# A recurrence, experts and an MLP on one core: the decay scan split in four and moved, outputs turned in place of decays, activations stored transposed

## The chip, the cores and the metric

The kernel runs on one core of one Trainium2 chip, all in float32. The time is the device time of one execution in microseconds, and the number compared is the median of the runs. TensorE (PE) multiplies matrices, VectorE (DVE), ScalarE (ACT) and GpSimd (POOL) work elementwise, SyncE (SP) here issues all DMAs. Each engine has its own queue and works through it in order; semaphores tie the queues together.

## The reference

Three stages follow each other. With B = 4 batches, H = 8 heads, S = 768 tokens and D = 40 channels, the first is a recurrence over tokens with a 40x40 state for each of 32 (batch, head) pairs:

```python
for t in range(S):
    y[:, :, t] = einsum('bhd,bhde->bhe', rt, state)
    Sa = einsum('bhde,bhe->bhd', state, at)
    state = state * wt[:, :, None, :] - einsum('bhd,bhe->bhde', Sa, bt) + einsum('bhd,bhe->bhde', vt, kt)
```

Its output, as x of 4 x 768 x 320, goes through four experts, each a causal softmax attention with head size 64 (queries, keys, values, softmax, output matrix); every token takes its two best experts, weighted by a softmax over their gate logits. The last stage is an MLP: `relu(x @ w_in)` gives 1024 features, the second 512 are normalised, mixed over tokens by a 768x768 matrix with a bias, multiplied by the first 512 and brought back to 320 by `w_out`.

## The kernel before

**The recurrence** (`recurrence`, lines 26 to 1176). Tokens are cut into 24 units of 128 (4 batches of 6 blocks), a unit into 4 chunks of 32. Heads are packed: q = 0 to 3 counts pairs of heads, x = 0, 1 the head of a pair, and channels of the two heads lie at partitions 0 to 39 and 64 to 103. Within a chunk the recurrence is written in matrix form, with decays divided out: keys are multiplied by the running products of decays towards the chunk's end (`s_ch`, a backward scan over w, `scan_s`, line 970), and `a` by the running products of decays from the chunk's start (`d_ch`, `scan_d`, line 988; its start values are reciprocals that `chunk_decays`, line 979, makes out of `dc_pos`). A triangular inverse per chunk is made by repeated squaring in five levels (`level`, `level_read`, `first_power`, `grams`).

The state is carried through each chunk by three hops (`hop` on TensorE, line 874; `chain` on VectorE, line 1103). Hop 0: TensorE L892 and L898 (`a` times state) into one bank, VectorE L1110 copies it to `g_tok`. Hop 1: TensorE L908, VectorE L1118 makes `vu_tok`. Hop 2: TensorE L920, VectorE L1126 adds the state (`state_sum`), L1140 multiplies it by the next chunk's decay into `state_z`, which the next chunk's L898 reads; GpSimd L458 (`decayed_state`) makes `state`, which the next L1126 adds. Twelve hops, 4 chunks of 3, are a beat, and a beat serves one unit.

Behind every hop each engine does a piece of work for other units; what stands where is written out by hand in the functions `between` (TensorE line 800, VectorE line 1071, SP line 297) and in the loops of GpSimd (line 478) and ScalarE (line 612). In beat u, r = u + 3, t = u + 2, v = u + 1, w = u - 1 and x = u - 2 are the units worked on:

- TensorE: chunk 0: `first_grams(t)`, `turn_states(w, 0)`, `turn_decays(v)` (L662: four blocks of `d_ch`) behind hop 0; `from_values(x, 2)` and a quarter of level 1 behind hop 1, the rest of it behind hop 2. Chunk 1: `turn_values(w)` and `from_states(x, 2)`, then half of level 0 and a quarter of level 2, then the rest of level 2. Chunk 2: `grams(t, 1)`, `turn_states(w, 1)`, `r_products(w)`, then level 0 and 3. Chunk 3: `turn_keys(v)`, `from_states(w, 0)` (L784), which waits for `rvu_read`, then `from_values` and level 4.
- VectorE: `scan_s(r)` at (0,0), that is chunk 0, hop 0; `first_power(t)` (0,1); `chunk_decays(r)` and `level_read(v, 1)` (0,2); `scan_d(r)`, first half (1,0); `y_read(x)` (1,1); `scan_d(r)`, second half (1,2); `keys_of_a(t)` and `level_read(v, 2)` (2,0); `r_read(w)` (2,1), which makes `rvu` (L1058); `level_read(v, 3)` (3,0); `level_read(t, 0)` (3,1); `level_read(v, 4)` (3,2).
- GpSimd: `scaled_keys(r)` (two instructions L421, `kb_ch`, which wait for `scan_s`), `decayed_state` 0, `first_factor(t)` (L411), `sorted_decays(r)`, `decayed_state` 1, `scaled_a(r)` (L447, `a_ch`, waits for both halves of `scan_d`), `decayed_state` 2 and 3.
- ScalarE: copies of what TensorE turned (among them `decays_read`, L558, `d_tok`), `spread_power` (L510), `copy_power`, `pad_a` (waits for `a_ch`).

The outputs of a unit gather in one PSUM bank by tokens. `y_read` (L1068) multiplies them by the turned decays `d_tok` into `y_tok`, and SP stores them in 16 DMAs of 10 KB a unit (`store`, L283) into `x_dram`, laid out token by feature.

In the last three units the product of the experts' output matrix and `w_in` (`fold`, L705, 12 steps of which each third is copied by ScalarE) is put between the hops.

**Experts and MLP** (`experts_and_mlp`, line 1177). It starts when `recurrence_done` holds. For each batch n: `turn_x(n)` (L1481, L1484: 18 transposes, six groups copied alternately by VectorE, L1793, and ScalarE, L1431) makes x^T, `values_and_gates(n)` (L1501, L1505), then the MLP's hidden layer and factors of batch n - 1, `queries_and_keys(n)`, and 12 steps of attention with the dense work of batch n - 1 between. SP loads the next batch's `x_tok` once `turn_x` is through.

## Time and profile before

| what | us |
|---|---|
| median of 3 runs | 1008.67 (1002.89 to 1014.07) |
| profiled execution | 1012.26 |
| its span, first to last instruction | 1010.4 |
| last g copy (L1110) of the recurrence starts | 487.8 |
| first turn of x (L1481) starts | 501.7 |

Busy share of the span: TensorE 96%, VectorE 51%, ScalarE 46%, GpSimd 24%. The mean granted clock of TensorE was 0.978 of full speed; 1.00 is 2.4 GHz and 0.50 is 1.2 GHz. A line number such as L898 is the line of the kernel that issued the instruction. In a timeline row a figure after x is a count: a row of `x8` gives the first start and the time to the last end of eight instructions, which overlap with what follows. A bracket gives the engine's idle time ahead of the row and what ended it.

### The profile page before, as it was taken

What the parts mean: (1) busy time and instruction counts of PE and PEld (TensorE: products, weight loads), DVE (VectorE), ACT (ScalarE), POOL (GpSimd) and SP (SyncE); (2) the same over time, 40 slices, a digit from 0 to 9 for tenths busy, and PEclk for the clock granted to TensorE, in tenths of its full rate; (3) what the DMA queues carried; (4) which work ended last, traced back from release to release, by engine and by line L of the source; (5) the groups of instructions that cost most, each with busy time, mean ns of one, the idle gap of its engine ahead of it and who ended that gap; (6) DMA issues with size and microseconds to landing.
All of it is one profiled execution on the core that took longest, in us unless ns stands there. A gap on an engine that the chain in (4) does not pass through costs nothing.

```text
span 1010.4 us, 36940 instructions
## 1 busy us (share of the span) xinstructions
PE 966.7 (96%) x15708; PEld 696.7 (69%) x15708; DVE 519.6 (51%) x1443; ACT 461.7 (46%) x1122; POOL 239.0 (24%) x344
## 2 busy tenths in 40 slices
PE   6989999999999999989998999999999999999998
PEld 4878888878888888877655755567545665556555
DVE  7578777778777787744335333322343223432130
ACT  6465655555555655643227443443434424344501
POOL 8345444344344344311000000100001000110011
PEclk8599999999999999988999999999999999999999
DMA  4244344344334334241150100002000000000001
GB/s 150 63 110 112 117 118 131 90 142 126 98 99 127 96 103 130 65 128 49 36 180 2 40 1 1 1 14 66 0 1 1 21 20 0 1 1 22 19 1 39
DMA packets 51539, 63.68 MB, mean 63 GB/s; under 512 B 27440, under 2 KB 37488, under 8 KB 51376
## 3 DMA queue, kind: packets, MB, share of 16 engines
q1 hardware_dynamic: 51376, 61.32, 20.5%
q8 instruction: 125, 2.05, 0.8%
q14 instruction: 38, 0.31, 0.1%
HBM read 53.42 MB, written 7.86 MB: 61 GB/s over the span
## 4 chain that ended last, share of the span: by engine, by line
PE 82%; DVE 11%; issue 4%; ACT 2%; DMA 1%; DVEq 0%
PE banks L1628 13%; PE banks L662 7%; PE banks L726 6%; PE banks L1567 5%; PE banks L1545 4%; PE banks L1519 4%; PE banks L1596 4%; PE banks L1640 4%; PE banks L1609 4%; PE banks L1579 4%; DVE state_z L1140 4%; PE banks L908 3%; PE banks L898 3%; PE banks L773 3%; PE banks L920 2%
## 5 line engine op out<-in xcount | busy, mean ns | idle before, releaser
L510 ACT ACTIVATE powers_z<-powers,parity 128x256 f32<-128x256 f32 x240 | 108.5, 500 | 172.3 <-DVE powers L1013 172.2
L726 PE MATMUL banks<-pq,powers_z 64*64 64x64 f32 (+1 forms) x3072 | 136.6, 228 | 11.7 <-issue 5.9
L1390 POOL TENSOR_TENSOR v_st<-v_st,u_t 128x384 f32<-128x384 f32 x32 | 32.0, 999 | 473.9 <-DVE v_st L1783 473.9
L1628 PE MATMUL banks<-w_st,v_n 128*128 128x384 f32 x384 | 139.0, 496 | 0.2 <-DVE v_n L1773 0.2
L726 PEld LDWEIGHTS banks<-pq,powers_z 64*64 64x64 f32 x3072 | 115.7, 142 | 17.6 <-issue 8.8
L458 POOL TENSOR_TENSOR state<-state_sum,dc 128x160 f32<-128x160 f32 x92 | 69.0, 750 | 184.9 <-DVE state_sum L1126 184.9
L1395 ACT ACTIVATE probs_t<-banks 128x512 f32<-128x512 f32 (+1 forms) x96 | 51.8, 543 | 122.4 <-PE banks L1567 122.4
L1628 PEld LDWEIGHTS banks<-w_st,v_n 128*128 128x128 f32 x384 | 67.5, 190 | 48.2 <-issue 10.8
L1118 DVE SCALAR_TENSOR_TENSOR vu_tok<-banks,minus,vz_tok 128x80 f32<-128x80 f32 x192 | 48.8, 296 | 73.7 <-PE banks L908 73.7
L1726 DVE CUSTOM_DVE_ANT_0 probs<-banks,hide 128x128 f32<-128x128 f32 (+5 forms) x96 | 56.0, 622 | 53.3 <-PE banks L1545 53.0
L1409 ACT ACTIVATE probs<-probs,neg_max 128x128 f32<-128x128 f32 (+5 forms) x96 | 63.3, 660 | 31.4 <-DVE neg_max L1726 31.3
L421 POOL TENSOR_TENSOR kb_ch<-w_all,s_ch 128x512 f32<-128x512 f32 x46 | 57.6, 1275 | 39.0 <-issue 34.4
L1748 DVE TENSOR_TENSOR o_t<-banks,share_t 128x256 f32<-128x256 f32 x24 | 10.2, 425 | 100.3 <-ACT share_t L1395 88.5
L1640 PE MATMUL banks<-w,v_st 128*128 128x320 f32 x192 | 57.6, 434 | 0.0
L1567 PE MATMUL banks<-ident,probs 128*128 128x128 f32 x336 | 54.1, 282 | 1.4 <-ACT probs_t L1395 1.4
L1567 PEld LDWEIGHTS banks<-ident,probs 128*128 128x128 f32 x336 | 38.1, 141 | 24.2 <-issue 15.1
L1545 PE MATMUL banks<-k_t,q_t 64*128 64x512 f32 (+3 forms) x256 | 50.1, 490 | 1.6 <-DVE k_t L1821 1.1
L1140 DVE TENSOR_TENSOR state_z<-state_sum,dc_side 128x320 f32<-128x320 f32 x92 | 49.9, 542 | 3.2
L1579 PEld LDWEIGHTS banks<-probs_t,vg 128*64 128x64 f32 x672 | 35.8, 137 | 20.6 <-issue 17.4
L1783 DVE TENSOR_TENSOR v_st<-banks,bias 128x384 f32<-128x384 f32 x32 | 17.8, 556 | 59.7 <-PE banks L1628 59.7
L1579 PE MATMUL banks<-probs_t,vg 128*64 128x128 f32 x672 | 47.5, 281 | 0.1
L662 PE MATMUL banks<-ident,state_z 104*128 104x104 f32 x384 | 45.6, 262 | 0.4 <-issue 0.4
(165 smaller groups left out, 1813.7 us busy)
## 6 DMA issues: line engine op xcount, KB each, us to landing
w_all<-decays_dram SPq DMA_DIRECT2D x48, 160.0 KB
w_all<-kb_ch_dram SPq DMA_DIRECT2D x48, 160.0 KB
vz_tok<-vz_tok_dram SPq DMA_DIRECT2D x24, 320.0 KB, 3.5
r_all<-rz_ch_dram SPq DMA_DIRECT2D x48, 160.0 KB
x_dram<-y_tok SPq DMA_DIRECT2D x384, 10.0 KB, 1.9
a_raw<-a_ch_dram SPq DMA_DIRECT2D x48, 80.0 KB
vc_tok<-vc_tok_dram SPq DMA_DIRECT2D x24, 160.0 KB, 3.9
r_all<-r_ch_dram SPq DMA_DIRECT2D x48, 80.0 KB
```

The lines of the kernel that those rows point to most:

```text
L421: pool.tensor_tensor(*keys_by_decays(u, a), ALU.mult).then_inc(kb_scaled, 1)
L458: pool.tensor_tensor(state[:, d % 2], state_sum[:, :, :], dc[:, v % 4, d].unsqueeze(2).to_broadcast([P, Q, D]), ALU.mult)\
L510: act.activation(powers_z[:, i, :, j, :], powers[:, i, :, :], ACT.Copy, scale=parity[:, j:j + 1])\
L662: return pe.transpose(to[:, 0:CHANNELS], src[0:CHANNELS], ident[0:CHANNELS, 0:CHANNELS])
L726: ins = pe.matmul(to[r, k * n:k * n + n], powers_z[r, i, k, :, :].rearrange("p j t -> p (j t)"), right, start=True, stop=True)
L1140: dve.tensor_tensor(to_z[:, :, :, 0:D], state_sum[:, :, :].unsqueeze(2).to_broadcast([P, Q, 2, D]), dc_side[:, v % 4, d].unsqueeze(3).to_b ...
L1409: act.activation(probs[:, s % 3, a, 0:width], probs[:, s % 3, a, 0:width], ACT.Exp, scale=-1.0, bias=neg_max[:, i, e:e + 1], accum_out=den ...
L1545: ins = pe.matmul(bank[2 * a + (j if width > 512 else s % 2)][:, 0:w], q_t[rows, p, i * P:i * P + P], k_t[rows, p, c:c + w], start=True, s ...
L1567: ins = pe.transpose(turn_bank(n, m)[:, x * P:x * P + P], src, ident[:, :])
L1579: ins = pe.matmul(bank[O_BANK][64 * a:64 * a + HD, p * P:p * P + P], vg[:, j, e * HD:e * HD + HD], probs_t[:, s % 2, a * (i + 1) + j, :], ...
L1628: ins = pe.matmul(bank[M_BANK + j % 2][:, 0:TH], v_n[:, i, d * P:d * P + P], w_st[:, i, t], start=(i == 0), stop=(i == BLOCKS - 1))
L1640: ins = pe.matmul(bank[M_BANK + i % 2][:, 0:F], gated[:, d, i * P:i * P + P], w_2[:, d, :], start=(d == 0), stop=(d == DT - 1))
```

## The change

`y_read`, `turn_decays` and `decays_read` go. In their place ScalarE copies a unit's outputs out of PSUM (`outputs_copied`), TensorE turns them (`turn_outputs`, three beats after the unit's own), ScalarE copies them back (`outputs_taken`), and GpSimd multiplies them by the untouched `d_ch` in four pieces (`decayed_outputs`), between `decayed_state` 2 and 3. `d_ch` gets seven buffers instead of three. The result is feature by token, so `x_dram` becomes [B, F, S], a unit is stored by 2 DMAs instead of 16, and the experts load x^T directly, in three DMAs a batch into one of two buffers; `turn_x` and its copies go. The loops run one or two beats longer at the end.

The decay scan is done in four parts of one chunk each, at (0,2), (1,1), (1,2) and (2,1), and `chunk_decays`, `level_read(v, 1)`, `first_power` and `r_read` change places; on TensorE level 0 and level 2 in chunk 1, on ScalarE `spread_power(t, 0)`, and on GpSimd `sorted_decays` and `first_factor` too. `square` shares the memory of `state_n`, and the last fold steps have banks of their own.

```diff
@@ SP
-            def store(u, c):
+            def store(u, x):
                 b, n = u // BLOCKS, u % BLOCKS
                 sp.wait_ge(y_done, at(u, y_done))
-                t = n * P + c * C
-                for q in range(Q):
-                    _, _, g, _ = place(c, q)
-                    sp.dma_start(x_out[b, t:t + C, q * X:q * X + X],
-                                 y_tok[rows32(g), u % 2, c, :, :].rearrange("p x d -> p (x d)"))\
-                        .then_inc(y_stored[u % 2], 16)
+                to = x_out[b].rearrange("(q x d) t -> x d q t", x=2, d=D)
+                sp.dma_start(to[x, :, :, n * P:n * P + P], y_ch[rows40(x), u % 2, :, :]).then_inc(y_stored[u % 2], 16)
@@ GpSimd
+            def decayed_outputs(u):
+                pool.wait_ge(y_taken, at(u, y_taken))
+                if u > 1:
+                    pool.wait_ge(y_stored[u % 2], at(u // 2 - 1, y_stored[u % 2]))
+                for c in range(NC):
+                    dst = y_ch[:, u % 2, :, c * C:c * C + C].rearrange("p (a b) t -> p b a t", a=2)[:, :, ::-1, :]
...
+                    pool.tensor_tensor(dst, y_raw[:, c * P:c * P + P].rearrange("p (b a t) -> p b a t", b=2, a=2),
+                                       d_ch[:, u % DECAYS, c * P:c * P + P].rearrange("p (b a t) -> p b a t", b=2, a=2),
+                                       ALU.mult).then_inc(y_done, 1)
...
                 if valid(u):
                     decayed_state(u, 0)
+                if valid(u + 3):
+                    sorted_decays(u + 3)
                 if valid(u + 2):
                     first_factor(u + 2)
-                if valid(u + 3):
-                    sorted_decays(u + 3)
...
                 if valid(u):
                     decayed_state(u, 2)
+                if valid(u - 3):
+                    decayed_outputs(u - 3)
+                if valid(u):
                     decayed_state(u, 3)
@@ ScalarE
-                copy(d_tok[:, v % 4].rearrange("p c x d -> p (c x) d"),
-                     bank[D_BANK][:, :].rearrange("p (k d) -> p k d", d=64)[:, :, 0:D]).then_inc(d_read, 1)
+            def outputs_copied(w):
+                act.wait_ge(y_ready, at(w, y_ready))
...
+                copy(y_tok[:, :, :, 0:D].rearrange("p c x d -> p (c x) d"),
+                     bank[Y_BANK][:, 0:NC * X].rearrange("p (k d) -> p k d", d=D)).then_inc(y_copied, 1)
+            def outputs_taken(w):
+                act.wait_ge(y_turned, at(w, y_turned))
...
+                copy(y_raw[0:CHANNELS, :], bank[Y_TURN_BANK][0:CHANNELS, :]).then_inc(y_taken, 1)
...
-                if valid(v):
-                    decays_read(v)
+                if valid(u - 3):
+                    outputs_taken(u - 3)
-                if valid(t):
-                    spread_power(t, 0)
                 if valid(v):
                     spread_power(v, 2)
                     copy_power(v, 1)
+                if valid(t):
+                    spread_power(t, 0)
                 if valid(w):
                     values_read(w)
+                if valid(x):
+                    outputs_copied(x)
@@ TensorE
-                        turn_decays(v)
+                    if valid(u - 3):
...
+                        turn_outputs(u - 3)
                 if (c, j) == (0, 1):
...
-                        pe.wait_ge(d_read, at(v, d_read))
+                        if valid(u - 3):
+                            pe.wait_ge(y_taken, at(u - 3, y_taken))
                         level(v, 1, 0, 2)
...
-                if (c, j) == (1, 1):
-                    if valid(t):
-                        level(t, 0, 0, 4)
-                    if valid(v):
-                        level(v, 2, 0, 2)
-                if (c, j) == (1, 2) and valid(v):
-                    level(v, 2, 2, N8)
+                if (c, j) == (1, 1) and valid(v):
+                    level(v, 2, 0, 4)
+                if (c, j) == (1, 2):
+                    if valid(v):
+                        level(v, 2, 4, N8)
+                    if valid(t):
+                        level(t, 0, 0, 4)
@@ VectorE
-            def scan_d(u, half):
+            def scan_d(u, first, last):
...
-                m = slice(half * W // 2, (half + 1) * W // 2)
...
+                m = slice(first * P, last * P)
+                dve.tensor_tensor_scan(d_ch[:, u % DECAYS, m], w_ch[:, u % 2, 1, m], d_start[:, m], 0.0, ALU.mult, ALU.add)\
+                    .then_inc(d_done, last - first)
...
                 if (c, j) == (0, 0) and valid(r):
                     scan_s(r)
+                if (c, j) == (0, 1) and valid(r):
+                    chunk_decays(r)
+                if (c, j) == (0, 2) and valid(r):
+                    scan_d(r, 0, 1)
+                if (c, j) == (1, 0):
                     if valid(v):
                         level_read(v, 1)
+                    if valid(t):
+                        first_power(t)
+                if (c, j) == (1, 1) and valid(r):
+                    scan_d(r, 1, 2)
                 if (c, j) == (1, 2) and valid(r):
+                    scan_d(r, 2, 3)
                 if (c, j) == (2, 0):
+                    if valid(v):
+                        level_read(v, 2)
                     if valid(t):
                         keys_of_a(t)
+                if (c, j) == (2, 1) and valid(r):
+                    scan_d(r, 3, 4)
+                if (c, j) == (3, 0):
+                    if valid(w):
+                        r_read(w)
                     if valid(v):
+                        level_read(v, 3)
@@ experts
-                    turn_x(n)
                     values_and_gates(n)
...
+    def load_x(self, sp, src, x_t, x_last, loaded):
+        F, TH = src.shape[0], self.S // 2
+        sp.dma_start(x_t[:, :, :], src[0:2 * P, :].rearrange("(k p) t -> p k t", p=P)).then_inc(loaded, 16)
+        for h in range(2):
+            sp.dma_start(x_last[h * self.LAST:h * self.LAST + self.LAST, :], src[F - self.LAST:F, h * TH:h * TH + TH])\
+                .then_inc(loaded, 16)
```

## Rows read from the trace of the kernel before

**Rows 1.** Windows view: stretch, its length, busy us of each engine, granted clock, DMA
```profile
71.00:429.00 358.00, 340.02 (x10427) 295.98 (x10418) 273.43 (x722) 204.46 (x495) 159.32 (x213) 1.00 0.39 112
429.00:461.00 32.00, 28.80 (x693) 25.04 (x685) 13.86 (x41) 13.32 (x34) 4.52 (x6) 0.79 0.41 117
...
568.00:1010.40 442.40, 438.79 (x2091) 262.33 (x2090) 137.44 (x420) 157.61 (x398) 31.95 (x32) 1.00 0.04 14
```

**Rows 2.** Timeline, TensorE, one beat (unit 15): start us, us, instructions
```profile
317.42 0.35 PE L898 MATMUL banks<-state_z,a_ch 128*32 128x80 f32 x8
...
318.92 0.52 PE L662 MATMUL banks<-ident,d_ch 104*128 104x104 f32 x4
319.37 0.43 PE L908 MATMUL banks<-g_tok,tz 64*64 64x40 f32 x8
...
322.25 0.35 PE L898 MATMUL banks<-state_z,a_ch 128*32 128x80 f32 x8 [0.41 <-DVE state_z L1140]
...
326.46 0.35 PE L898 MATMUL banks<-state_z,a_ch 128*32 128x80 f32 x8
...
329.13 0.43 PE L908 MATMUL banks<-g_tok,tz 64*64 64x40 f32 x8
...
330.26 0.35 PE L920 MATMUL banks<-vu_tok,kb_tok 64*40 64x40 f32 x14
...
331.62 0.35 PE L898 MATMUL banks<-state_z,a_ch 128*32 128x80 f32 x8
...
332.76 0.48 PE L784 MATMUL banks<-state_n,r_all 128*32 128x80 f32 x16
...
335.66 0.35 PE L898 MATMUL banks<-state_z,a_ch 128*32 128x80 f32 x8
```

**Rows 3.** Timeline, VectorE, the same beat
```profile
321.41 0.79 DVE L1140 TENSOR_TENSOR state_z<-state_sum,dc_side 128x320 f32<-128x320 f32 x1
...
323.53 0.67 DVE L996 TENSOR_TENSOR_SCAN d_ch<-w_all,d_start 128x256 f32<-128x256 f32 x1
...
326.32 0.94 DVE L996 TENSOR_TENSOR_SCAN d_ch<-w_all,d_start 128x256 f32<-128x256 f32 x1
...
329.60 0.51 DVE L1118 SCALAR_TENSOR_TENSOR vu_tok<-banks,minus,vz_tok 128x80 f32<-128x80 f32 x2 [0.91 <-PE banks L908]
330.03 0.68 DVE L1058 TENSOR_TENSOR rvu<-banks,upper 128x512 f32<-128x512 f32 x1
...
331.07 0.49 DVE L1140 TENSOR_TENSOR state_z<-state_sum,dc_side 128x320 f32<-128x320 f32 x1
332.03 0.24 DVE L1110 COPY g_tok<-banks 128x80 f32<-128x80 f32 x1 [0.47 <-PE banks L898]
```

**Rows 4.** Timeline, GpSimd and ScalarE, the same beat
```profile
319.34 2.51 POOL L421 TENSOR_TENSOR kb_ch<-w_all,s_ch 128x512 f32<-128x512 f32 x2 [1.66 <-issue]
...
319.77 0.44 ACT L502 ACTIVATE d_tok<-banks 128x320 f32<-128x320 f32 x1
...
327.40 1.28 POOL L447 TENSOR_TENSOR a_ch<-a_raw,d_ch 128x512 f32<-128x512 f32 x1 [0.68 <-issue]
```

**Rows 5.** Timeline, GpSimd and VectorE, the first beat
```profile
33.73 2.50 POOL L421 TENSOR_TENSOR kb_ch<-w_all,s_ch 128x512 f32<-128x512 f32 x2 [2.46 <-issue]
...
35.19 1.40 DVE L1140 TENSOR_TENSOR state_z<-state_sum,dc_side 128x320 f32<-128x320 f32 x1
```

**Rows 6.** Chain of waits in order of time, chunk 1 of unit 12
```profile
267.11 0.72 PE banks L726 x24
```

**Rows 7.** Timeline, TensorE, end of the recurrence and start of batch 2
```profile
500.63 0.48 PE L784 MATMUL banks<-state_n,r_all 128*32 128x80 f32 x16
...
503.85 0.60 PE L1501 MATMUL banks<-w_vg,x_t 128*128 128x260 f32 x2
...
692.42 0.38 PE L1481 MATMUL banks<-ident,x_tok 128*128 128x128 f32 x2
...
694.82 0.39 PE L1501 MATMUL banks<-w_vg,x_t 128*128 128x260 f32 x1
```

More of the change, by code:

```diff
@@ L175, in recurrence @@
         y_ready = sem("y_ready_r", 1)
-        y_done = sem("y_done", 1)
-        y_stored = [sem("y_stored%d" % i, 16 * 16) for i in range(2)]
+        y_pads = sem("y_pads", 0)
+        y_copied = sem("y_copied", 1)
+        y_turned = sem("y_turned", 1)
+        y_taken = sem("y_taken", 1)
+        y_done = sem("y_done", NC)
+        y_stored = [sem("y_stored%d" % i, 2 * 16) for i in range(2)]
         fold_loaded = sem("fold_loaded", 0)
@@ L315, in between @@
                         load_r(u, j - 1, False)
-                if valid(u - 2) and c >= 2 and j > 0:
-                    store(u - 2, 2 * (c - 2) + j - 1)
+                if valid(u - 4) and c == 2 and j > 0:
+                    store(u - 4, j - 1)
             def load_first(u):
@@ L352, in _ @@
             load_first(1)
-            for u in range(-2, UNITS + 2):
+            for u in range(-2, UNITS + 4):
                 for c in range(NC):
@@ L477, in _ @@
             scaled_a(2)
-            for u in range(UNITS + 1):
+            for u in range(UNITS + 3):
                 if valid(u + 3):
@@ L611, in _ @@
             spread_power(0, 4)
-            for u in range(UNITS + 1):
-                r, t, v, w = u + 3, u + 2, u + 1, u - 1
+            for u in range(UNITS + 3):
+                r, t, v, w, x = u + 3, u + 2, u + 1, u - 1, u - 2
                 if valid(u):
@@ L939, in _ @@
             turn_keys(0)
-            pe.wait_ge(d_read, at(0, d_read))
             level(0, 1)
@@ L950, in _ @@
             level(1, 0, 4, N8)
-            for u in range(UNITS + 2):
+            for u in range(UNITS + 3):
                 for k in range(12):
@@ L1246, in experts_and_mlp @@
         vg_loaded, qk_loaded, consts = shared.vg_loaded, shared.qk_loaded, shared.consts
-        per[shared.x_loaded], start[shared.x_loaded] = 16, 0
         x_loaded = shared.x_loaded
+        for i in range(2):
+            per[x_loaded[i]], start[x_loaded[i]] = shared.X_LOADS, 0
         w_late = sem("w_late", 0)
-        x_turned = sem("x_turned", BLOCKS)
-        x_read_dve = sem("x_read_dve", BLOCKS // 2)
-        x_read_act = sem("x_read_act", BLOCKS // 2)
         v_ready = sem("v_ready", BLOCKS)
@@ L1524, in queries_and_keys @@
                         pe.matmul(bank[V_BANKS[j % 4]][:, 0:TH], w_qk[rows, which, NK - 1, q * P:q * P + P],
-                                  shared.x_last[rows, :], start=False, stop=True).then_inc(qk_ready, 1)
+                                  x_last[n % 2][rows, :], start=False, stop=True).then_inc(qk_ready, 1)
             def scores(n, s):
@@ L1649, in _ @@
             pe.wait_ge(consts, shared.CONSTS)
-            after_recurrence(pe)
+            for done, count in shared.banks_done:
+                pe.wait_ge(done, count)
             for n in range(B + 1):
                 if n < B:
-                    turn_x(n)
                     values_and_gates(n)
```

181 lines of the change are left out of this document (71 added, 110 removed).

## The prediction

> **What bounds the kernel now.** I read the stretches first [rows 1]. From 71 to 429 us the kernel runs 19 beats of the recurrence (units 2 to 20), 358.00 / 19 = 18.84 us each, with TensorE busy for 340.02 of 358.00 us at full clock. From 568 us on TensorE is busy for 438.79 of 442.40 us: there its work alone is the time, and what is taken from its queue comes off the end one for one. The recurrence looks just as full, but one undisturbed beat in order of time shows something else [rows 2]. Its four chunks, from the first L898 to the next, take 4.83, 4.21, 5.16 and 4.04 us, 18.24 in all. In chunk 2 hop 1 starts at 329.13, hop 2 at 330.26 (+1.13), and the next L898 at 331.62 (+1.36). These 2.49 us are a chain: TensorE L908, VectorE `vu_tok` (329.60), TensorE L920, VectorE `state_sum` and `state_z` (331.07, 0.49 us, so till 331.56), TensorE L898 0.06 later [rows 2, 3]. TensorE's fillers between hops only use this time up. The rest of a chunk, L898 to L908 (4.21 - 2.49 = 1.72 us in chunk 1, 326.46 to 329.13 is 2.67 in chunk 2), is TensorE work. So a chunk is (fillers behind the first hop) + 2.49, and only chunk 0 has more: 1.95 (317.42 to 319.37) + 2.49 = 4.44 against 4.83, the 0.39 being mostly a `state_z` of 0.79 instead of 0.49. The mean beat is 0.6 us over the clean one, in TensorE stops with no releaser.
>
> That 0.79 is the important row. `kb_ch` on GpSimd runs from 319.34 for 2.51 us, to 321.85; `state_z` begins at 321.41 and ends at 322.20, 0.35 after it [rows 3, 4]. In the first beat `state_z` begins at 35.19, and `kb_ch`, from 33.73, ends at 36.23; `state_z` takes 1.40 and ends at 36.59, again about 0.35 behind [rows 5]. It has two inputs in SBUF and doesn't advance until GpSimd's instruction is over.
>
> The Trainium skill, SBUF — State Buffer, section Who interferes with whom, says the same as a rule: a VectorE instruction with two SBUF inputs and a GpSimd instruction that reads SBUF exclude each other, whoever issues first holds for the whole instruction. It speaks against this change as those rows do; by its words the price in chunk 2 below is the same 0.63, and its "first" leaves open who goes between two queued GpSimd instructions, which is the second rival.
>
> **The change, part by part, for a beat.**
>
> *Chunk 0.* TensorE turns four blocks of outputs instead of four of decays: 0.52 us for four of 104 columns at 318.92 [rows 2]; these move 128, so 0.43 x 128/104 is about +0.1. ScalarE copies 104x512 instead of 128x320 (0.44 at 319.77 [rows 4]), about 0.15 more, and level 1 waits for it as it did for `d_read`. On VectorE `dc_pos` and the reciprocal stand where `n_t` and the turn stood. All of this is ahead of `state_z`, whose end is set by `kb_ch`; `dc_pos` can only slip between the halves of `kb_ch` and push the second by 0.05. I take +0.05 (bounds -0.3, if `state_z` came free of `kb_ch`, to +0.8, rival B).
>
> *Chunk 1.* `level_read` 1 and `first_power` now follow hop 0 one after the other, and ahead of them the first part of the scan waits for `state` on GpSimd. TensorE's level 2, which before stood behind level 0 in hop 1, now comes first and needs ScalarE's spread and copy of just that result. Four VectorE pieces of about 0.4 us from the g copy (0.59 behind L898) end at about the 2.19 us (1.72 + 0.47) when `vu_tok` is due, and the ScalarE steps end some 2.5 us behind L898, with half of a level (16 of the matmuls that run 24 in 0.72 us [rows 6], 0.5) to do before L920 is due at 2.85. That is 3.0 against 2.85: +0.15 (bounds 0 and +0.4). The GpSimd order change (`sorted_decays` ahead of `first_factor`) has room.
>
> *Chunk 2.* `scaled_a` waits for all four parts of the scan. Before, the last half (326.32 for 0.94) ended at 327.26 and `a_ch` ran at 327.40 for 1.28 us, with no two-input piece of VectorE beside it [rows 3, 4]. Now part 3 stands behind `vu_tok` of chunk 2: it starts 0.43 behind 329.60, at 330.03, where `rvu` starts now. 256 elements take 0.67 [rows 3], so 128 take some 0.40, to 330.43. `a_ch` follows 0.14 later, 330.57 to 331.85. `state_z` is due at 331.07 and would end 0.35 behind 331.85, at 332.20, not 331.56: +0.63. TensorE has nothing else: L892 is done, and L898 waits for `state_z`. Queued behind `a_ch` on GpSimd is `state` for the next `state_sum`, over 3 us away, and behind it the four pieces of `decayed_outputs`, some 0.4 us each by `a_ch`'s rate (1.28 for 512), over before the next `state_z`; they are free unless that rate is wrong by a factor of two. ScalarE's `pad_a` waits too, but ends before its next piece is due. Bounds of the step: 0 (VectorE gets in first) and +0.9 (what the first beat's 1.40 shows over 0.49). I take +0.63. Stops of TensorE in this chunk, about 0.2 of the 0.6 us per beat, then fall in idle time: -0.2.
>
> *Chunk 3.* `rvu` (0.68 us) moves from hop 1 of chunk 2 to behind hop 0 here, and TensorE's L784 needs it. The g copy (332.03) starts 0.41 behind L898 and takes 0.24, `rvu` starts 0.08 before it ends, as it does behind `vu_tok`, and ends at 0.41 + 0.16 + 0.68 = 1.25; TensorE sees it 0.06 later, at 1.31, and L784 starts at 332.76 - 331.62 = 1.14 now [rows 2, 3]: +0.17. The level read behind it is late by the same 0.68, and so are ScalarE's spread and level 4, which had most of that to spare: +0.08. Together +0.25 (bounds +0.1 and +0.5).
>
> Sum of a beat: 0.05 + 0.15 + 0.63 - 0.20 + 0.25 = +0.88 us. All of it applies where unit u + 3 exists, 21 beats (0 to 20): **+18.5 us**. The three left have only chunk 3's part, hidden in the first loads and folds: 0.
>
> *Stores and loads.* 16 stores a beat become 2, on a DMA system busy for 0.39 of the time [rows 1]; SP waits for `y_done` of the unit before last, long over. No hop waits for a store now, so 0; if the stops without releaser are instruction loads behind those stores, up to 0.6 x 19 = 11 us could come back. Nothing in these rows ties them together.
>
> *Tail.* Two more turns (0.5 each) stand in TensorE's queue, one partly in a wait, and one unit of pipeline is added: the last L784 ends at 501.1 [rows 7]; from there +0.7 (the two turns), then ScalarE's copy 0.5, the turn 0.6, the copy back 0.6, with hand-overs 0.4: matmuls L1501 at 503.9 to 504.3, where they start at 503.85 now, since the 18 turns of x go. **+0.3** (0 to +1.5). GpSimd's last products and the stores lie beside batch 0's values.
>
> *Expert stage.* For batches 1 to 3 the turns of x go too, and x^T is loaded a batch ahead into the other buffer, so no wait replaces them: 692.42 to 694.82 is 2.40 for batch 2, batch 3 is like it, and batch 1 has the 18 turns without the 0.4 of stops, 2.0 [rows 7]. The six ScalarE and six VectorE copies of each were beside. **-6.8** (bounds -6.0 and -7.2).
>
> *Start.* One turn and its wait go, under 0.7 us: -0.3.
>
> Total 18.5 + 0.3 - 6.8 - 0.3 = +11.7. The profiled execution took 1012.26 (span 1010.40 and 1.86 around it), which would give 1024.0. That execution is 3.6 us over the median of 1008.67, so the forecast is 1008.67 + 11.7 = **1020.4 us**.
>
> **Rivals.**
>
> *A, not slower.* VectorE's `state_z` is not held by `a_ch` (it gets in first, or the part scan ends so late that `a_ch` issues behind it), and the hand-overs of chunks 1 and 3 fit. Then a beat changes by +0.05 to -0.3 and the expert stage decides: 1008.67 - 6.8 + 0 = 1001.9, down to 995 if the 0.39 of chunk 0 goes as well, 21 x 0.3. It decides once a beat's gain of time is under 0.3 us. For it: the pieces are clearly spaced so that none stands ahead of a `state_sum`. Against: `a_ch` would have to start half a microsecond later than `scan` + 0.14.
>
> *B, slower still.* `dc_pos` (two SBUF inputs) arrives at about 320.35, in the first half of `kb_ch`, and is passed by the second half too. Then it ends at 321.9, the reciprocal behind it 0.3 later, `state_sum` follows, 0.36 to `state_z`, and 0.49: the end is at 323.05 and not 322.20, +0.8. 21 x 0.8 = 17, so 1037. Against: `state_z` at 321.41 gets in ahead of the `state` that GpSimd issues next.
>
> *C, the clock.* In the stretch from 429 to 461 the granted clock was 0.79, after a stop of TensorE of 3 us [rows 1]. More idle in every beat could bring such falls in mid-recurrence. One like that is worth 4 to 8 us: 1025 to 1030. Against: it stays at 1.00 through all smaller stops of 71 to 429.
>
> **Chances.** Forecast (chunk 2 is stretched, the rest as summed, 1011 to 1029) 0.55, A 0.25, B 0.10, C 0.10. Its own range is 1011 to 1029, and the range for 8 in 10 takes in most of A and part of B: 999 to 1032. A change under 1% is about what a measurement of this kernel can't tell from none, here 998.6 to 1018.8. Slower by over 1%: 0.55 x 0.6 + 0.17 of B and C = 0.50. Faster by over 1%: 0.4 of A plus returned stops, 0.14. Within: 0.36.
>
> **What would show it.** In the profile of after: `state_z` of chunk 2 at about 1.1 us and `a_ch` beginning before it; a clean beat near 19.1; `dc_pos` under 0.4; L784 some 0.2 later in chunk 3; no L1481, and L1501 right behind the last turn of a batch. I am wrong if `state_z` stays at 0.49 in chunks 1 to 3, if the mean beat is under 18.8, or if x^T is waited for.

## The result, and the profile after

The change makes the kernel slower by a little: 1014.40 us (median of 20 runs, 1010.38 to 1018.99) after 1004.86 us (20 runs, 999.86 to 1017.30), a ratio of 1.0083 with a 95% interval of 1.0058 to 1.0107. The ratio is that of the means of the runs, without two slow ones of the kernel before (1015.61 and 1017.30 us): 1014.41 to 1006.07, which is +8.3 us, where +11.7 was forecast; the two medians above differ by 9.5. The bound of 1% lies inside the interval, so by the chances given it counts as the middle case, near its upper edge. A second comparison of the two, a2 below, gave 1.0046 (1.0012 to 1.0081).

The profiled execution after took 1013.90 us (span 1011.50), only 1.6 us more than the one before. The windows view of the kernel after, with its columns as in [rows 1]; the first row holds units 2 to 20, the second the rest of the recurrence:

```profile
71.90:441.20 369.30, 338.98 (x10409) 293.82 (x10408) 288.60 (x743) 212.43 (x513) 181.63 (x286) 1.00 0.39 108
441.20:510.00 68.80, 64.13 (x1492) 47.08 (x1492) 28.11 (x83) 27.65 (x67) 16.31 (x30) 1.00 0.28 76
```

The same 19 beats took 358.00 us before and take 369.30 now, +11.3, and TensorE's busy time in them even fell a little: the time added is idle. That it shows as 1.6 us in the whole has its reason in the execution before. Its timeline (TensorE) and its windows behind the same point:

```profile
444.85 0.62 PE L726 MATMUL banks<-pq,powers_z 64*64 64x64 f32 x15 [2.98 <-issue]
```

```profile
446.00:461.00 15.00, 15.00 (x280) 13.05 (x276) 5.58 (x17) 6.51 (x17) 1.51 (x2) 0.54 0.23 63
```

TensorE stood for 2.98 us with no releaser (the trace names nothing that ended the wait, and such a wait is marked "issue"), and its granted clock then lay near half (0.54, so mostly the 1.2 GHz level) for some 14 us. A second execution of the same kernel has neither. From start to end, after less before, the two profiled executions differ by +1.3 (to unit 2), +11.3 (units 2 to 20), -4.8 (units 21 to 23, that stop and slow stretch), +2.1 (from the last L940, before L898, to batch 0's first matmul), -8.9 (expert stage), in all the 1.1 of span, but for rounding. Of the -8.9, 2.0 + 2.4 + 2.4 = 6.8 are the turns of x; nearly all the rest lies in batch 0, where before has a second half-clock stretch. Executions at full clock give both disturbed stretches as they are without it. The kernel before takes 52.2 us for units 21 to 23 in its second execution (b4 below), and b1 and b2, which have the same last units, 53.1 and 52.2, where after takes 54.0: +0.9 to +1.9. The expert stage of b1 and b2, the same as before's, takes 504.7 where after's takes 497.7: -7.0. The sum then is 1.3 + 11.3 + 0.9 (or 1.9) + 2.1 - 7.0 = +8.6 to +9.6 us, against the 8.3 and 9.5 above. The first term is scatter: the start of unit 2 lies between 67.5 and 72.3 us over all the traces.

A clean beat is below the sum of the lengths that the four chunks have when nothing disturbs them, the mean beat is the mean of units 2 to 20, and the difference of the two is called the stops. It holds TensorE's stops without releaser in the main, and whatever else disturbs single beats. One undisturbed beat of the kernel after, unit 15, in order of time. TensorE:

```profile
325.48 0.35 PE L940 MATMUL banks<-state_z,a_ch 128*32 128x80 f32 x8
...
330.31 0.35 PE L940 MATMUL banks<-state_z,a_ch 128*32 128x80 f32 x8 [0.25 <-DVE state_z L1175]
...
334.62 0.35 PE L940 MATMUL banks<-state_z,a_ch 128*32 128x80 f32 x8
...
340.40 0.35 PE L940 MATMUL banks<-state_z,a_ch 128*32 128x80 f32 x8 [0.68 <-DVE state_z L1175]
...
341.71 0.48 PE L821 MATMUL banks<-state_n,r_all 128*32 128x80 f32 x16
...
344.62 0.34 PE L940 MATMUL banks<-state_z,a_ch 128*32 128x80 f32 x8
```

VectorE and GpSimd, chunk 0 first and then chunk 2 with the head of chunk 3:

```profile
327.40 2.50 POOL L424 TENSOR_TENSOR kb_ch<-w_all,s_ch 128x512 f32<-128x512 f32 x2 [1.66 <-issue]
...
328.41 0.30 DVE L1024 TENSOR_TENSOR dc_pos<-w_all,s_ch 128x16 f32<-128x16 f32 x1
...
329.55 0.70 DVE L1175 TENSOR_TENSOR state_z<-state_sum,dc_side 128x320 f32<-128x320 f32 x1
...
338.19 0.42 DVE L1036 TENSOR_TENSOR_SCAN d_ch<-w_all,d_start 128x128 f32<-128x128 f32 x1
...
338.74 1.27 POOL L450 TENSOR_TENSOR a_ch<-a_raw,d_ch 128x512 f32<-128x512 f32 x1 [3.97 <-issue]
...
339.23 1.12 DVE L1175 TENSOR_TENSOR state_z<-state_sum,dc_side 128x320 f32<-128x320 f32 x1
...
340.62 1.70 POOL L463 TENSOR_TENSOR y_ch<-y_raw,d_ch 128x128 f32<-128x128 f32 x4
...
340.98 0.68 DVE L1098 TENSOR_TENSOR rvu<-banks,upper 128x512 f32<-128x512 f32 x1
```

Read beside [rows 2 to 4]: the chunks take 4.83, 4.31, 5.78 and 4.22 us here (medians 4.82, 4.31, 5.79, 4.21, in all 19.13), before 4.83, 4.20, 5.16, 4.04 (18.23). In chunk 2 the last part of the scan ends at 338.61, `a_ch` starts 0.13 later and ends at 340.01; `state_z`, begun at 339.23, ends at 340.35, 0.34 behind it, and L940 has idled 0.68 us for it. Before, `a_ch` ran at the head of chunk 2 ([rows 4], 327.40, which is 0.94 behind its L898, where it now begins 4.12 behind L940), and no VectorE piece with two SBUF inputs stood beside it. The head of chunk 3, L940 to L821, is 1.31 us, where it was 1.14.

The waits view (TensorE, 71 to 420 us; us in total, times, longest) counts what the mean beat holds. Before:

```profile
PE banks L898 <- DVE state_z L1140: 3.3, 9, 0.4
PE banks L726 <- issue: 2.9, 6, 1.0
```

After:

```profile
PE banks L940 <- DVE state_z L1175: 16.1, 32, 0.7
PE banks L762 <- ACT pq L525: 4.2, 18, 0.2
PE banks L762 <- issue: 2.1, 3, 1.1
```

The wait for `state_z` grows from 3.3 to 16.1 us, a new one of 0.24 per beat stands in chunk 1 (L762 for ScalarE's copy of the powers), and all stops without releaser ("issue") together fall from 10.0 to 2.6 us.

### The profile page after: what moved, and what is told of

Its sections match the earlier page's. It is cut to its first block, busy times and chain, and to the rows that moved or that the text cites. A ratio compares the mean times of both kernels' runs of the same rounds, so it can differ in the third digit from the quotient of the medians.

```text
span 1011.5 us, 36574 instructions
## 1 busy us (share of the span) xinstructions
PE 949.0 (94%) x15636; PEld 680.0 (67%) x15636; DVE 529.0 (52%) x1437; ACT 464.3 (46%) x1122; POOL 271.6 (27%) x442
## 2 busy tenths in 40 slices
DMA packets 39855, 63.62 MB, mean 63 GB/s; under 512 B 9616, under 2 KB 24784, under 8 KB 39696
## 4 chain that ended last, share of the span: by engine, by line
PE 76%; DVE 12%; ACT 5%; issue 5%; DMA 1%; DVEq 0%; ACTq 0%
PE banks L1642 13%; PE banks L762 8%; PE banks L1581 5%; PE banks L1559 4%; PE banks L1593 4%; PE banks L1533 4%; PE banks L1610 4%; PE banks L1654 4%; PE banks L1623 4%; PE banks L695 4%; DVE state_z L1175 4%; PE banks L810 3%; PE banks L962 3%; PE banks L940 3%; PE banks L712 2%
## 5 line engine op out<-in xcount | busy, mean ns | idle before, releaser
L762 PE MATMUL banks<-pq,powers_z 64*64 64x64 f32 (+1 forms) x3072 | 132.9, 225 | 14.5 <-ACT pq L525 8.8
L762 PEld LDWEIGHTS banks<-pq,powers_z 64*64 64x64 f32 x3072 | 113.0, 138 | 22.1 <-ACT powers_z L533 15.4
L1642 PEld LDWEIGHTS banks<-w_st,v_n 128*128 128x128 f32 x384 | 67.5, 190 | 48.2 <-issue 10.8
L1175 DVE TENSOR_TENSOR state_z<-state_sum,dc_side 128x320 f32<-128x320 f32 x92 | 62.9, 684 | 3.2
L525 ACT ACTIVATE az_ch<-a_ch 64x512 f32<-64x512 f32 x48 | 30.2, 629 | 56.0 <-POOL a_ch L450 53.9
L940 PE MATMUL banks<-state_z,a_ch 128*32 128x80 f32 x768 | 33.5, 247 | 21.3 <-DVE state_z L1175 19.3
L450 POOL TENSOR_TENSOR a_ch<-a_raw,d_ch 128x512 f32<-128x512 f32 x23 | 29.2, 1270 | 90.1 <-issue 81.4
L1036 DVE TENSOR_TENSOR_SCAN d_ch<-w_all,d_start 128x128 f32<-128x128 f32 (+1 forms) x90 | 50.5, 562 | 0.2
```

Of the source, the lines that this page charges most:

```text
L762: ins = pe.matmul(to[r, k * n:k * n + n], powers_z[r, i, k, :, :].rearrange("p j t -> p (j t)"), right, start=True, stop=True)
L940: ins = pe.matmul(to[rows32(g), 0:X], a_ch[:, u % 4, cols(blk)], state_z[:, u % 2, c, q, :, 0:D], start=False, stop=True, skip_group_check ...
L1175: dve.tensor_tensor(to_z[:, :, :, 0:D], state_sum[:, :, :].unsqueeze(2).to_broadcast([P, Q, 2, D]), dc_side[:, v % 4, d].unsqueeze(3).to_b ...
L1642: ins = pe.matmul(bank[M_BANK + j % 2][:, 0:TH], v_n[:, i, d * P:d * P + P], w_st[:, i, t], start=(i == 0), stop=(i == BLOCKS - 1))
```

## The experiments

The theory: the last part of the scan, behind `vu_tok` of chunk 2, moves `a_ch` beside `state_z`, which does not advance until GpSimd's instruction is over; the rest is small. The rivals: the order of TensorE's work or the stores make the time. All ratios below are to the kernel before, from the runs beside the kernel in question. The times of b1, b2, b3, e2 and e3 are single runs, so what they say rests on the trace; single runs of before lie between 998.75 and 1020.42 us.

**e1: the scan undone.** The kernel after, with the last two parts of the scan in one piece behind hop 2 of chunk 1:

```diff
                 if (c, j) == (1, 2) and valid(r):
-                    scan_d(r, 2, 3)
+                    scan_d(r, 2, 4)
...
-                if (c, j) == (2, 1) and valid(r):
-                    scan_d(r, 3, 4)
```

> The changed kernel with the last part of the decay scan back at chunk 1, hop 2 (one scan of 256 there), so a_ch is released a hop and a half earlier. Theory: state_z of chunk 2 is back at 0.49, chunk 2 at 5.16 instead of 5.79, chunks 0, 1 and 3 stay at 4.82, 4.31 and 4.21, a clean beat is 18.5; 21 beats x 0.63 = 13 us less, of which stops of TensorE that were hidden in chunk 2's idle time give 2 to 4 back: about 1003 to 1005, or 0.998 to 1.001 of the kernel before. Rival (chunk 2 grew because of what stands on VectorE in its hops): no more than half of that.

Measured: 1005.76 us (1002.71 to 1006.60, 10 runs), ratio to before 0.9991 (0.9965 to 1.0018). The timeline:

```profile
328.13 1.28 POOL L450 TENSOR_TENSOR a_ch<-a_raw,d_ch 128x512 f32<-128x512 f32 x1 [0.68 <-issue]
...
331.92 0.49 DVE L1173 TENSOR_TENSOR state_z<-state_sum,dc_side 128x320 f32<-128x320 f32 x1
```

`a_ch` is back at the head of chunk 2, `state_z` is 0.49 us, chunk 2 is 5.16 as before, and the other chunks stay at the change's lengths (4.82, 4.31, 4.21). One part of four, moved by two hops, takes the change's loss away; what is then left in the other chunks and the tail the expert stage makes up for. The stops are 0.38 us here.

**b1, b2, b3: the same in the kernel before.** One added wait ahead of `scaled_a(u + 3)` in GpSimd's loop, and nothing else of the change:

```diff
                 if valid(u + 3):
+                    pool.wait_ge(u_read, at(u, u_read, 6))
                     scaled_a(u + 3)
```

b2 waits for `state_ready` of chunk 2 (`at(u, state_ready, 3)`), b3 for `state_summed` (`at(u, state_summed, 3)`).

> The kernel before; GpSimd's a_ch product waits in addition for vu_tok of chunk 2, nothing else moves. My theory (state_z of chunk 2 can't advance while a_ch runs): a_ch starts some 0.65 us behind the start of vu_tok and runs 1.28, so state_z of chunk 2 takes about 0.8 us instead of 0.49 and chunk 2 of a clean beat (L898 to L898) 5.5 instead of 5.16. Rival 1 (the later scan on VectorE, not a_ch, costs the time in the changed kernel): chunk 2 stays at 5.16 here, since VectorE's order is untouched. Rival 2 (GpSimd is simply behind with its queue): state_z stays at 0.49 and a wait for the product state shows in chunk 3.

> As the run before, but a_ch waits for hop 2 on TensorE (L920 of chunk 2). Theory: a_ch starts at about 1.6 us behind hop 1 (L908), before state_z (1.94), and ends at 2.9: state_z takes about 1.3 us, chunk 2 about 6.0 us (+0.8). Rival 1: chunk 2 stays at 5.16. A beat then is near 19.1 clean, the total some 15 us over the kernel before.

> As before, but a_ch waits for state_sum of chunk 2, so it is issued just behind state_z. Theory (who issues first holds): state_z of chunk 2 stays at 0.49 and chunk 2 at 5.16 although a_ch comes latest of the three; a_ch itself takes about 1.7 us. The time comes back elsewhere: ScalarE's pad_a waits for a_ch and holds up the spread for level 4, so chunk 3 grows from 4.04 to about 5.1. A theory of plain overlap (both slowed while both run) expects state_z of 0.8 or more here too.

Measured: 1006.90, 1015.20 and 1034.57 us, beside 1006.82 for before (13 runs). Timelines of b1, b2 and b3:

```profile
350.06 1.27 POOL L447 TENSOR_TENSOR a_ch<-a_raw,d_ch 128x512 f32<-128x512 f32 x1 [3.48 <-DVE vu_tok L1119]
...
351.03 0.65 DVE L1141 TENSOR_TENSOR state_z<-state_sum,dc_side 128x320 f32<-128x320 f32 x1
```

```profile
357.71 1.26 POOL L447 TENSOR_TENSOR a_ch<-a_raw,d_ch 128x512 f32<-128x512 f32 x1 [4.04 <-PE banks L921]
358.02 1.30 DVE L1141 TENSOR_TENSOR state_z<-state_sum,dc_side 128x320 f32<-128x320 f32 x1
...
359.37 0.35 PE L899 MATMUL banks<-state_z,a_ch 128*32 128x80 f32 x8 [0.85 <-DVE state_z L1141]
```

```profile
367.92 0.49 DVE L1141 TENSOR_TENSOR state_z<-state_sum,dc_side 128x320 f32<-128x320 f32 x1
...
367.97 1.57 POOL L447 TENSOR_TENSOR a_ch<-a_raw,d_ch 128x512 f32<-128x512 f32 x1 [4.40 <-DVE state_sum L1127]
...
371.84 0.30 PE L727 MATMUL banks<-pq,powers_z 64*64 64x32 f32 x4 [0.97 <-ACT powers_z L511]
```

`state_z` ends 351.68 - 351.33 = 0.35 us behind `a_ch` in b1 and 359.32 - 358.97 = 0.35 in b2, whatever time it began, so its own length (0.65, 1.30) is only how late `a_ch` was. Chunk 2 follows: 5.41 and 5.96. In b3 `a_ch` issues 0.05 us after `state_z`: now `state_z` is untouched (0.49, chunk 2 5.16) and `a_ch` takes 1.57 instead of 1.27. Here who issues first holds the other. The Trainium skill, SBUF — State Buffer, section Who interferes with whom, describes such an exclusive hold between VectorE and GpSimd; the three rows agree. `rvu`, with one of its inputs in PSUM, stands beside GpSimd's `y_ch` in the rows of the kernel after (340.98) and keeps its 0.68 us.

b3 is no gain all the same. ScalarE's padding of `a_ch` (1.28 us) follows that late, the powers behind it are late for TensorE by 0.97 us, and chunk 3 goes from 4.04 to 4.95. Its windows view, for mid-recurrence and for chunk 0 of unit 8, where TensorE had waited those 0.97 us in the chunk ahead:

```profile
70.00:429.00 359.00, 332.05 (x9701) 289.75 (x9693) 255.11 (x674) 190.02 (x459) 147.71 (x199) 0.94 0.38 107
```

```profile
192.58:198.71 6.13, 5.99 (x148) 5.33 (x148) 3.70 (x10) 2.87 (x8) 3.26 (x4) 0.72 0.25 64
```

The granted clock of mid-recurrence is 0.94, where it is 1.00 in before and after: this is the forecast's rival C, seen in a kernel whose wait is longer (0.97 against 0.68 us) and not in the change itself. It falls in chunk 0: in unit 8 it is 0.50, the 1.2 GHz level, from 193 to 196 us, TensorE being busy, and the chunk takes 6.13 us in place of 4.83. Over the 19 beats chunk 0 has 0.72 in nine (6.07 to 6.13 us), 0.50 in one (7.44 us, behind a stop of 2.46), and 1.00 in the other nine (4.83 to 5.11 us), though the wait of chunk 3 stands ahead of nearly all. A clean beat, 4.83 + 4.20 + 5.16 + 4.95 = 19.14, is 0.91 us over before's, which makes 19 us over 21 beats; the mean beat (20.23 against 18.84) gives 29, and the run 28. The clock's part is most of the rest.

**e2: `a_ch` in two halves.** The kernel after, with

```diff
-                pool.tensor_tensor(a_ch[:, u % 4, :], a_raw[:, u % 2, :], d_ch[:, u % DECAYS, :], ALU.mult)\
-                    .then_inc(a_scaled, 1)
+                for i in range(2):
+                    m = slice(i * W // 2, (i + 1) * W // 2)
+                    ins = pool.tensor_tensor(a_ch[:, u % 4, m], a_raw[:, u % 2, m], d_ch[:, u % DECAYS, m], ALU.mult)
+                ins.then_inc(a_scaled, 1)
```

> The changed kernel, only a_ch made by two GpSimd instructions of 256 elements instead of one of 512. Theory (state_z is held to the end of the GpSimd instruction that runs when it issues, and then goes first): the first half ends about 0.65 us behind its start, some 0.15 us behind the start of state_z, so state_z takes about 0.5 to 0.6 us instead of 1.12 and chunk 2 5.2 to 5.3 instead of 5.79. Rival (state_z waits until a_ch is made, or GpSimd's two instructions run through): 1.1 or more and 5.79.

Measured: 1004.48 us. The timeline:

```profile
351.31 1.67 POOL L452 TENSOR_TENSOR a_ch<-a_raw,d_ch 128x256 f32<-128x256 f32 x2 [3.97 <-issue]
...
351.80 0.58 DVE L1177 TENSOR_TENSOR state_z<-state_sum,dc_side 128x320 f32<-128x320 f32 x1
...
355.28 0.30 PE L764 MATMUL banks<-pq,powers_z 64*64 64x32 f32 x4 [0.27 <-ACT powers_z L535]
```

`state_z` gets in between the halves: 0.58 us instead of 1.12, chunk 2 5.25 instead of 5.79. The second half now waits for it (1.67 for both instead of 1.27), the padding comes 0.4 late, and chunk 3 gives back 0.20 (4.41). The clean beat is 18.79. How much of the GpSimd instruction is left when `state_z` issues is the price of the collision, as one `a_ch` of 512 shows against two of 256.

**e3: `rvu` a hop earlier.** The kernel after, with `r_read` at hop 2 of chunk 2:

```diff
-                if (c, j) == (3, 0):
-                    if valid(w):
-                        r_read(w)
-                    if valid(v):
-                        level_read(v, 3)
+                if (c, j) == (2, 2) and valid(w):
+                    r_read(w)
+                if (c, j) == (3, 0) and valid(v):
+                    level_read(v, 3)
```

> The changed kernel with r_read (rvu) behind hop 2 of chunk 2 instead of hop 0 of chunk 3. My theory: L821 no longer waits for rvu, and level 4 gets its input earlier: chunk 3 from 4.21 to about 4.04, the rest unchanged, 0.17 x 22 = 3.7 us. Rival (chunk 3's 0.17 comes from GpSimd's four output products or from the level read alone): 4.21 stays.

Measured: 1004.20 us, and in the timeline:

```profile
333.56 0.34 PE L940 MATMUL banks<-state_z,a_ch 128*32 128x80 f32 x8 [0.68 <-DVE state_z L1174]
...
334.70 0.48 PE L821 MATMUL banks<-state_n,r_all 128*32 128x80 f32 x16
```

L821 stands 1.14 behind L940 again and chunk 3 takes 4.04: the 0.17 of this chunk was `rvu` and nothing else. The tail, from the last L940 to batch 0, goes from 18.55 to 17.53 as well (below). By the clean beat (18.96 for 19.13) and the tail that is 3.6 + 1.0 us; the rest of the single run's 10 is scatter, 3.8 of it in the start (unit 2 begins at 68.1 us, after 72.0).

**e4 and e8: sixteen stores a unit.** The kernel after with as many stores as before, in e4 of 40 rows of 256 bytes, in e8 of 20 rows of 512 bytes (`y_stored` counts 16 * 16 in both). e4:

```diff
-                sp.dma_start(to[x, :, :, n * P:n * P + P], y_ch[rows40(x), u % 2, :, :]).then_inc(y_stored[u % 2], 16)
+                for q in range(Q):
+                    for h in range(2):
+                        sp.dma_start(to[x, :, q, n * P + h * 64:n * P + h * 64 + 64],
+                                     y_ch[rows40(x), u % 2, q, h * 64:h * 64 + 64]).then_inc(y_stored[u % 2], 16)
```

e8 has in its place

```python
                        sp.dma_start(to[x, 20 * h:20 * h + 20, q, n * P:n * P + P],
                                     y_ch[64 * x + 20 * h:64 * x + 20 * h + 20, u % 2, q, :])\
                            .then_inc(y_stored[u % 2], 16)
```

> The changed kernel with each unit's outputs stored by 16 DMAs of 40 x 256 bytes instead of 2, about as many packets as the kernel before sends. It tells where TensorE's shorter stops without releaser come from (mean beat minus clean beat: 0.60 us before, 0.31 after). If the stores' packets cause them, they come back: mean beat over clean beat by 0.5 to 0.7, some 4 to 6 us slower than the changed kernel. If the idle time of the stretched chunk hides them, they stay at 0.3 and the total at 1.008 of before.

> The changed kernel with 16 stores a unit that carry 20 rows of 512 bytes each, so as many DMAs as in the run with many stores, but no more packets than the changed kernel. If packets made that run's stops (0.59), they stay at 0.3 here and the time is that of the changed kernel; if the number of DMAs that SP issues makes them, they are 0.5 to 0.6 again and the time is 5 us above it.

Measured: e4 1022.78 us (10 runs), ratio to before 1.0140 (1.0098 to 1.0182); e8 1021.61 us (10 runs), 1.0113 (1.0070 to 1.0156). Both clean beats are 19.13, chunk by chunk those of the change. The mean beat is 0.59 (e4) and 0.69 (e8) over the clean one, where the change has 0.31 and, in a repeat of it, 0.33. In the waits view of e4, TensorE's stops without releaser begin

```profile
PE banks L765 <- issue: 2.1, 3, 1.1
PE banks L937 <- issue: 2.0, 1, 2.0
```

and come to 6.7 us in 71 to 420 (e8 6.4), after the change's 2.6. So fourteen more DMAs a unit, with nothing else altered, bring TensorE stops back. How many is less sure: e4 has one stop of 2.0 us and e8 one of 2.5, with a half-clock stretch behind it, and without the longest beat of each trace the stops are 0.41 and 0.42 us a beat, where the change has 0.26 and its repeat 0.29. It does not go by the number of packets: the changed kernel has 39,855, e4 50,898, e8 only 43,218. In the time, e8 is 4.6 us over the repeat of the changed kernel in the same series (means of 10 runs each, 95% interval 1.1 to 8.2); the ratios' intervals overlap by a little.

The stores are not the whole of it either. Sorted by both, TensorE's stops without releaser in 71 to 420 us are, with two stores a unit and idle time in every beat, 2.6 (the change), 2.5 (its repeat), 2.3 (e3) and 1.3 (e2); with sixteen stores and idle time 6.7, 6.4 and 5.6 (b2); with two stores and little idle time 3.6 (e1), 5.6 and 7.1 (e6 and e7 below); with sixteen and little idle time 10.0 and, in a second execution, 7.0 (before) and 9.4 (b1). Idle time hides stops and more DMAs go with more of them; how the change's 0.29 divides between the two stays open.

**The two kernels once more**, unchanged, to see how far such figures repeat.

> The changed kernel once more, for a second trace and a time beside the runs below: chunks of a clean beat again 4.82, 4.31, 5.79 and 4.21; the stops without releaser (mean beat minus clean beat, 0.31 in the first trace) tell how far that number scatters between executions, 0.25 to 0.4 if it belongs to the kernel.

> The kernel before once more, one look: stops of 0.55 to 0.65 us a beat if the 0.60 of the first trace belongs to the kernel, 0.3 to 0.6 if it is scatter; the half-clock stretch at 446 to 460 us, and the stop of 3 us before it, absent, if that belonged to the one execution.

Measured: 1015.95 us (10 runs, 1.0046 as above) and, in one run, 1007.98. Clean beats again 19.13 and 18.23, stops 0.33 (0.31 in the first execution) and 0.61 (0.61). The clean beat repeats to 0.01 us, the stops to 0.02. The tail does not: it takes 20.05 us in a2, where the first execution has 18.55, at a granted clock of 0.91 in a2 and 1.00 in the first. In b4 it is 16.42, as before.

**e6 and e7: what is best.** e6 is the kernel after with the edits of e1 and e3, and with `kb_ch`'s second half behind `decayed_state(u, 0)`:

```diff
-            def scaled_keys(u):
+            def scaled_keys(u, then=None):
...
                 for a in range(2):
+                    if a == 1 and then is not None:
+                        then()
                     pool.tensor_tensor(*keys_by_decays(u, a), ALU.mult).then_inc(kb_scaled, 1)
...
-                    scaled_keys(u + 3)
-                if valid(u):
+                    scaled_keys(u + 3, then=lambda: decayed_state(u, 0))
+                elif valid(u):
                     decayed_state(u, 0)
```

e7 is e6 with ScalarE's last `folded(3)` moved from unit `UNITS` to behind `outputs_taken` one unit later.

> The changed kernel with three edits: the last scan part back at chunk 1, hop 2; r_read behind hop 2 of chunk 2; and the second half of the keys' product on GpSimd behind the product state of chunk 0, so that it no longer holds state_z of chunk 0. Theory: chunks 4.45, 4.31, 5.16 and 4.04, clean beat 17.96 against 19.13: 21 x 1.17 = 24.6 us less than the changed kernel, of which some 5 us come back as stops: 993 to 996, or 0.990 of the kernel before. If the hold of chunk 0 isn't by kb_ch, chunk 0 stays at 4.82 and the total is about 1000.

> The kernel with the three edits, and in addition ScalarE copies the last fold step only after it has taken unit 22's turned outputs. In the changed kernel GpSimd's products of unit 22 ended at 513.04, ScalarE's last copy began at 513.13 and the experts' first matmul at 513.83. Theory: the last copy then waits for the turn alone (0.75 us behind it is 512.4 in that trace), so the stretch from the last L940 to the experts is 0.7 us shorter than in the kernel with three edits (17.51), 16.8; the total 0.7 us less, too little to tell by time, 0.989 to 0.991 of the kernel before.

Measured: e6 998.54 us (10 runs), ratio to before 0.9902 (0.9862 to 0.9943); e7 998.40 (6 runs), 0.9877 (0.9836 to 0.9918). The timeline of e6, chunk 0:

```profile
334.14 0.49 DVE L1174 TENSOR_TENSOR state_z<-state_sum,dc_side 128x320 f32<-128x320 f32 x1
```

and of e7, ScalarE and TensorE at the end of the tail:

```profile
495.74 0.60 ACT L527 ACTIVATE y_raw<-banks 104x512 f32<-104x512 f32 x1 [0.80 <-PE banks L801]
...
496.43 3.75 PE L1514 MATMUL banks<-w_vg,x_t 128*128 128x260 f32 x16 [0.73 <-issue]
```

With `state_z` no longer held by GpSimd in an undisturbed beat, the clean beat of both is 4.62 + 4.31 + 5.16 + 4.04 = 18.13, 1.00 under the change's. Few beats are so clean: the median of e6's chunk 0 is 4.98 us. Chunk 0 ends 0.17 over the 4.45 that the same arithmetic as in the other chunks gives: the turn of 128 columns and TensorE's wait for `y_raw` stand in it, which is why the 17.96 expected was missed, and with it the 993 to 996 us. The mean beats are 18.65 and 18.75: more than half a microsecond goes back to stops. e7's tail is 16.69 us where e6's is 17.54; 0.8 us is less than the two comparisons can tell apart in the medians, so the trace alone shows it. These kernels beat both others, before by about 1%.

## Why the prediction was right or wrong, point by point

**Direction and size.** Slower was forecast, by 11.7 us; 8.3 was measured, inside the range of 999 to 1032. The half of the chances stood at over 1%, since the likeliest case lay itself at 1.2%. The beats were forecast too dear by 5.9 us, the tail and the last three units too cheap by about 3, as told below; that these errors partly cancel, and the total is off by only 3.4, is luck.

**Chunk 2, +0.63 a beat: measured +0.63.** `state_z` was forecast at about 1.1 us with `a_ch` beginning before it, and is 1.12 with `a_ch` 0.49 ahead. e1, b1, b2 and e2 show the cause. Rival A (VectorE gets in first) fell: `a_ch` issues 0.13 behind the scan, as the half microsecond that A wanted was not there.

**Chunk 3, +0.25: measured +0.17.** The `rvu` term, 0.17, is exact (e3). The 0.08 added for the level behind it was not there: ScalarE's slack covered it.

**Chunk 1, +0.15: measured +0.10**, and the waits view has a new wait in it, 0.24 us of L762 for ScalarE's copy of the powers. That this wait is the 0.10 was not tried by itself.

**Chunk 0, +0.05: measured -0.01.** `dc_pos` slips between the halves of `kb_ch` in most units (0.30 us, under the 0.4 named). But rival B's picture, passed by both halves, is real where `dc_pos` comes a little late. Unit 4 of the kernel after:

```profile
112.75 2.50 POOL L424 TENSOR_TENSOR kb_ch<-w_all,s_ch 128x512 f32<-128x512 f32 x2
...
114.04 1.24 DVE L1024 TENSOR_TENSOR dc_pos<-w_all,s_ch 128x16 f32<-128x16 f32 x1
...
116.33 0.34 PE L940 MATMUL banks<-state_z,a_ch 128*32 128x80 f32 x8 [0.64 <-DVE state_z L1175]
```

The first half ended at about 114.00, the second had issued when `dc_pos` came at 114.04, and 16 elements took 1.24 us. In steady state it comes at 1.01 behind `kb_ch`, here at 1.29. Past the first beat only this unit and the one at 231.12 have it at over 1.1 us (three units in a2), so B is worth 1 to 2 us of the whole and not 17.

**Stops, -0.20: measured -0.29.** The sign was right and the reason half right: idle in chunk 2 hides stops. The sentence that a return of stops tied to the stores had nothing in these rows for it missed that fewer stores could also take stops away, to which e4 and e8 point.

**The sum of a beat** is then -0.01 + 0.10 + 0.63 + 0.17 - 0.29 = +0.60 and not +0.88: over 21 beats +12.6 and not +18.5. This is the term that was mis-sized, by some 6 us, in small parts that all erred to the slow side.

**The last three units, 0: measured +0.9 to +1.9** (54.0 us, in a2 53.5, against 52.2, 53.1 and 52.2 in b4, b1 and b2). The forecast put chunk 3's part there as hidden. It is not: unit 22's chunk 3 takes 4.22 for b4's 4.05, and chunk 0 of unit 23 takes 4.43 where before and the kernels made from it take 4.12 or 4.13. What makes the latter was not tried.

**Tail, +0.3: measured +2.1** (18.55 us from the last L940 to batch 0, before 16.42). This step failed, and lies outside its own bounds of 0 to +1.5. In order of time, the kernel after:

```profile
496.58 0.48 PE L821 MATMUL banks<-state_n,r_all 128*32 128x80 f32 x16 [0.96 <-DVE rvu L1098]
...
510.18 0.60 ACT L525 ACTIVATE w_oi<-banks 128x512 f32<-128x512 f32 x1 [4.89 <-PE banks L741]
...
511.35 1.69 POOL L463 TENSOR_TENSOR y_ch<-y_raw,d_ch 128x128 f32<-128x128 f32 x4 [8.90 <-ACT y_raw L525]
...
513.13 0.60 ACT L525 ACTIVATE y_raw<-banks 104x512 f32<-104x512 f32 x1 [1.53 <-POOL y_ch L463]
...
513.83 3.53 PE L1515 MATMUL banks<-w_vg,x_t 128*128 128x260 f32 x15 [1.47 <-issue]
```

Three causes make 2.1 us, about the 1.8 that were missed. First, `rvu` in chunk 3 of the last unit: no other work of TensorE stands there any more, so it idles 0.96 us for it, and the hop behind it begins 1.72 us after L940 (497.00 - 495.28) where it began after 0.71 (488.14 - 487.43): +1.0. The forecast had this part "hidden in the first loads and folds"; e3 takes `rvu` a hop earlier and its tail is shorter by just 1.0. Second, there is one `y_raw` buffer. ScalarE takes unit 22's outputs late, since the last fold copy (510.18) is ahead of them; GpSimd's four products on them end at 513.04, and only then is unit 23's copy allowed, though its turn was over at 511.74 + 0.62 = 512.36: +0.8. The forecast put "GpSimd's last products" beside batch 0's values, which is true of the last unit and not of the one before it. e7 moves the fold copy, `y_raw` follows TensorE at once, and the tail goes from e6's 17.54 to 16.69. Third, the two turns cost 1.0 instead of 0.7 (from L898 or L940 of the last chunk to the last L784 or L821, 15.2 for 13.2, of which 1.0 is `rvu`'s). The hand-overs of 0.4 in all were right.

**Expert stage, -6.8: measured -7.0** at full clock (497.7 us for the 504.7 of b1 and b2). TensorE's timeline at the start of batch 2:

```profile
698.34 0.44 PE L1581 MATMUL banks<-ident,share_b 128*128 128x128 f32 x2
698.62 1.26 PE L1515 MATMUL banks<-w_vg,x_t 128*128 128x260 f32 x5
```

No turn of x stands between, where [rows 7] had 2.40 us, and x^T is not waited for.

**Start, -0.3**, was not resolved: up to unit 2 the profile shows +1.3, which holds units 0 and 1, worth 1.2 to 1.8 by the beats above, and which scatters by up to 5 us between executions. **Rival C** did not come: 1.00 from 71.9 to 510 us.

## What to carry to other kernels

An instruction of VectorE with two SBUF inputs on the critical path is to be looked at together with GpSimd's order: a GpSimd piece of 1.27 us that was early and harmless adds 0.63 us to every beat when its data are made two hops later, and 0.81 when it issues closer ahead (b2). When long pieces of one engine are moved "out of the way", follow the consumer of the last one, on whatever engine, and see what stands beside it then; splitting that consumer helped, and moving one of four parts back helped more. A pipeline made one stage deeper needs its buffers checked at the drain, where the producer of the unit before the last still holds them.
